# First-unit order of loads, TensorE, ScalarE and VectorE rewritten, with products of zeros ahead of the first scores

## The reference

```python
scores = scale * np.matmul(q, k.transpose(0, 1, 3, 2))          # batch 2, heads 8, seq 576, head_dim 64
mask_plain = (rel >= 0) & (rel < window)                        # window 32, heads 0..3
mask_dil = (rel >= 0) & (rel < window * dilation) & (rel % dilation == 0)
scores = scores - np.max(scores, axis=-1, keepdims=True)        # masked scores are -1e9
attn = np.exp(scores); attn = attn / (np.sum(attn, axis=-1, keepdims=True) + 1e-09)
x = np.matmul(attn, v)                                          # then as 1152 tokens x 512
for e in range(4):                                              # d_ff 1024
    out += p[:, e:e + 1] * (np.maximum(x @ w1[e], 0.0) @ w2[e])
h = out @ w_in                                                  # d_ff 2048
g = (a0 + a1*h + a2*h**2 + a3*h**3) / (1 + |b0||h| + |b1|h**2 + 1e-6)
return g @ w_out
```

## Time and profile before

| | us |
|---|---|
| median of 3 runs | 648.47 (646.71 to 650.09) |
| the profiled execution | 646.93 |
| its span, first to last instruction | 645.1 |
| PE busy | 633.8 |
| DVE / ACT / POOL busy | 387.2 / 319.1 / 268.9 |

### The profile page before, as it was taken

How to read it: one execution, slowest core, us unless ns; L and a number is a source line. 1 busy time by engine, 2 the same in 40 slices (tenths; PEclk the granted TensorE clock), 3 DMA queues, 4 the chain that set the end, 5 groups by cost and what they waited for, 6 DMA issues and landing times.

```text
span 645.1 us, 10644 instructions
## 1 busy us (share of the span) xinstructions
PE 633.8 (98%) x4004; PEld 563.4 (87%) x4004; DVE 387.2 (60%) x755; ACT 319.1 (49%) x742; POOL 268.9 (42%) x283
## 2 busy tenths in 40 slices
PE   6999999999999999999999999999999999999998
PEld 5788888988898889888898989889989998899996
DVE  4435352865665456234446325438988888889896
ACT  4874553333421343221443212336887777877774
POOL 4675112028860686300785100335722576732221
PEclk9999999999999999999999999999999999999999
DMA  9834220002130022100132100111530000001011
GB/s 305 260 92 131 62 73 1 2 33 67 66 98 2 34 99 98 34 2 1 42 109 80 33 1 1 59 41 49 162 149 1 1 0 2 2 0 50 2 49 50
DMA packets 20532, 37.68 MB, mean 58 GB/s; under 512 B 3392, under 2 KB 4032, under 8 KB 20480
## 3 DMA queue, kind: packets, MB, share of 16 engines
q1 hardware_dynamic: 20480, 36.99, 17.6%
HBM read 34.62 MB, written 2.36 MB: 57 GB/s over the span
## 4 chain that ended last, share of the span: by engine, by line
PE 94%; DMA 2%; ACT 1%; DVE 1%; issue 0%; SPq 0%; DVEq 0%; ACTq 0%
PE banks L739 46%; PE banks L655 24%; PE banks L713 20%; PE banks L627 2%; DMA scratch<-in_qk_dil 1%; PE banks L596 1%; PE banks L606 1%; DMA scratch<-in_qk_plain 1%; PE banks L775 1%; DVE h_lo L1262 0%; DVE acc L1168 0%; DVE acc L1163 0%; PE banks L615 0%; ACT scratch L856 0%; ACT w_hi L909 0%
## 5 line engine op out<-in xcount | busy, mean ns | idle before, releaser
L739 PE MATMUL banks<-w_hi,h_hi 128*128 128x512 f32 x432 | 171.6, 397 | 0.1
L739 PE MATMUL banks<-w_lo,h_hi 128*128 128x512 f32 x432 | 170.6, 395 | 0.0
L739 PE MATMUL banks<-w_hi,h_lo 128*128 128x512 f32 x429 | 169.9, 396 | 0.0
L1481 POOL TENSOR_TENSOR w_lo<-raw,w_hi 128x512 fp32r<-128x512 f32 x32 | 41.4, 1317 | 157.3 <-ACT w_hi L909 157.3
L655 PE MATMUL banks<-x_hi,w_hi 128*128 128x384 f32 (+1 forms) x320 | 104.9, 328 | 0.0
L655 PE MATMUL banks<-x_lo,w_hi 128*128 128x384 f32 (+1 forms) x320 | 102.5, 320 | 0.0
L655 PE MATMUL banks<-x_hi,w_lo 128*128 128x384 f32 (+1 forms) x320 | 102.3, 320 | 0.0
L1255 DVE TENSOR_TENSOR stage<-banks,stage 128x320 f32<-128x320 f32 (+1 forms) x120 | 54.1, 455 | 77.9 <-PE banks L713 75.0
L739 PEld LDWEIGHTS banks<-w_hi,h_lo 128*128 128x128 f32 x429 | 80.5, 188 | 19.3
L739 PEld LDWEIGHTS banks<-w_hi,h_hi 128*128 128x128 f32 x432 | 81.2, 188 | 14.6 <-issue 0.4
L739 PEld LDWEIGHTS banks<-w_lo,h_hi 128*128 128x128 f32 x432 | 81.2, 188 | 14.5
(11 more groups left out here) (116 smaller groups left out, 1240.4 us busy)
## 6 DMA issues: line engine op xcount, KB each, us to landing
raw<-in_weights SPq DMA_DIRECT2D x24, 512.0 KB, 3.6
raw<-in_weights SPq DMA_DIRECT2D x32, 256.0 KB, 2.7
raw_last<-in_weights SPq DMA_DIRECT2D x16, 256.0 KB, 5.5
scratch<-in_v SPq DMA_DIRECT2D x16, 192.0 KB, 4.0
scratch<-in_qk_dil SPq DMA_DIRECT2D x8, 320.0 KB, 5.2
out_t<-acc SPq DMA_DIRECT2D x9, 256.0 KB, 2.1
scratch<-in_qk_plain SPq DMA_DIRECT2D x8, 272.0 KB, 4.6
scratch<-in_qk_rest SPq DMA_DIRECT2D x2, 256.0 KB, 2.8
```

Source lines behind the costliest of these rows:

```text
L739: last = nc.tensor.matmul(sum_bank(k, t), h[:, cols], w[:, f, :], start=f == 0 and i == 0, stop=f == FC - 1 and i == 2)
L1481: last = nc.gpsimd.tensor_tensor(w1_lo[:, 2 * p + c].rearrange("p a b -> p (a b)"), raw1[:, c], w1_hi[:, 2 * p + c].rearrange("p a b -> p ...
```

## The change

All of it lies ahead of the steady loop, in the first unit.

- Loads: all query/key loads of blocks 0 to 3 come first, then all their value loads; the loads of blocks 4 to 7 are put among the eight weight loads. So `load_v(4)`, which waits for `values(0)`, stands ahead of `load_raw(4)`, and `load_v(5)` ahead of `load_raw(6)`. The three small loads (`prob`, `a_sb`, `b_sb`) come behind `load_v(7)`.
- PE: `fill` now multiplies a tile of zeros, which DVE sets in its first instruction, so it doesn't need the identity. Ten such products stand ahead of `scores(0)`, 28 more in five places (`FILLERS`); before there were 12 in three places. `turn(0)` comes ahead of `scores(4)`, and `values(3)` ahead of the whole `inner_product(0, 0)`. Chunks 1 and 3 are cut in two halves around a turn, not 3 to 1.
- DVE: block 0 is masked and reduced in two halves (`first_block`), so that ACT's exponentials of the first half can begin after the first. `mask(2)` comes ahead of `invert(0)`, and `mask(3)` ahead of `invert(1)`. DVE makes the high part of four inner weight chunks, no longer two.
- ACT: `exponentials(3)` comes ahead of `take_turned(1)`; `exponentials(4)` is no longer split around `attention_hi(2)` but stands behind `attention_hi(3)`; no `high_w1` ahead of `high(0, 0)`.

```diff
-FILLERS_FIRST = 4
-FILLERS = (3, 0, 5, 0)
+FILLERS = (10, 4, 12, 6, 3, 3)
...
-            def fill(w, n):
-
-                if w >= 2:
-                    pe.wait_ge(xa_lo, w - 1 if w < PAIRS else w)
+            def fill(bank, n):
+
                 for _ in range(n):
-                    nc.tensor.matmul(value_bank(w)[:, 0:P], ident[:, :], ident[:, :], start=True, stop=True)
+                    nc.tensor.matmul(bank[:, 0:P], zeros, zeros, start=True, stop=True)
...
+            pe.wait_ge(zeros_set, 1)
+            fill(turned_bank(0), FILLERS[0])
             scores(0)
...
-            def exponentials(w, part=None):
-                act.wait_ge(maxed, w + 1)
-                rows, part = soft_of(w), part or range(columns(w))
-                for n in part:
+            def exponentials(w):
+                if w == 0:
+                    act.wait_ge(first_maxed, 1)
+                else:
+                    act.wait_ge(maxed, w + 1)
+                rows = soft_of(w)
+                for n in range(columns(w)):
+                    if w == 0 and n == stacks(0):
+                        act.wait_ge(maxed, 1)
...
             def high_w1(c):
 
                 act.wait_ge(raw_in[c], 16)
+                act.wait_ge(w1_hi_done, 4)
...
+            def first_block():
+
+                dve.wait_ge(scored, 1)
+                dve.wait_ge(masks_made, 1)
+                m, n = start_mask.rearrange("p s c -> p (s c)"), stacks(0)
+                for half, done in ((0, first_maxed), (1, maxed)):
+                    part = slice(half * n, half * n + n)
+                    nc.vector.scalar_tensor_tensor(out=soft_of(0)[:, part, :].rearrange("p s c -> p (s c)"),
+                                                   in0=score_banks(0)[:, half, :], scalar=-SCALE, in1=m,
+                                                   op0=ALU.mult, op1=ALU.subtract)\
+                        .then_inc(first_masked if half == 0 else masked, 1)
...
+                    nc.vector.tensor_reduce(neg_max[:, 0, part], soft_of(0)[:, part, :], axis=AX.X, op=ALU.min)\
+                        .then_inc(done, 1)
...
+            nc.vector.memset(zeros, 0.0).then_inc(zeros_set, 1)
...
-            mask(0)
-            maximum(0)
+            first_block()
             mask(1)
             maximum(1)
+            mask(2)
             dve.wait_ge(small_set, 1)
             invert(0)
-            mask(2)
             maximum(2)
+            mask(3)
             invert(1)
-            mask(3)
             maximum(3)
```

More of the change, by code:

```diff
@@ L286, in build @@
         rest_mask = carve(TK)
+        zeros = carve(P)
         soft = carve(SOFT * 4 * TK).rearrange("p (s n c) -> p s n c", s=SOFT, c=TK)
@@ L313, in build @@
         prob_step = sem("prob_step")
+        zeros_set = sem("zeros_set")
         scored = sem("scored")
+        first_masked = sem("first_masked")
+        first_maxed = sem("first_maxed")
         masked = sem("masked")
@@ L528, in _ @@
                 load_qk(w)
-                if w:
-                    load_v(w - 1)
-            load_v(PAIRS - 1)
+            for w in range(PAIRS):
+                load_v(w)
+            load_raw(0)
             load_qk(PAIRS)
-            for c in range(FC):
-                load_raw(c)
-                if c == 2:
-                    load_qk(PAIRS + 1)
+            load_raw(1)
+            load_raw(2)
+            load_qk(PAIRS + 1)
+            load_raw(3)
+            load_v(PAIRS)
+            load_raw(4)
+            load_raw(5)
+            load_qk(PAIRS + 2)
+            load_v(PAIRS + 1)
+            load_raw(6)
+            load_raw(7)
+            load_qk(PAIRS + 3)
+            load_v(PAIRS + 2)
+            load_v(PAIRS + 3)
             sp.dma_start(prob[:, :, 0:MOE], probs).then_inc(prob_in, 16)
@@ L539, in _ @@
             sp.dma_start(b_sb[:, :], b.partition_broadcast(P)).then_inc(ab_in, 16)
-            for w in range(PAIRS, 2 * PAIRS):
-                if w >= PAIRS + 2:
-                    load_qk(w)
-                load_v(w)
             for w in range(2 * PAIRS, 3 * PAIRS):
@@ L777, in turn_x2 @@
                 last.then_inc(x2_turned, 1)
+            pe.wait_ge(zeros_set, 1)
+            fill(turned_bank(0), FILLERS[0])
             scores(0)
             scores(1)
-            pe.wait_ge(ident_made, 1)
-            fill(0, FILLERS_FIRST)
+            fill(turned_bank(0), FILLERS[1])
             scores(2)
             scores(3)
+            fill(turned_bank(0), FILLERS[2])
+            pe.wait_ge(ident_made, 1)
+            turn(0)
+            fill(turned_bank(1), FILLERS[3])
+            turn(1)
+            fill(value_bank(0), FILLERS[4])
+            values(0)
+            turn(2)
             scores(4)
-            turn(0)
-            turn(1)
-            fill(0, FILLERS[0])
-            values(0)
+            fill(value_bank(1), FILLERS[5])
             values(1)
-            turn(2)
-            fill(2, FILLERS[2])
+            turn(3)
             values(2)
-            turn(3)
-            inner_product(0, 0, range(DC - 1))
             values(3)
-            inner_product(0, 1, range(DC - 1))
-            inner_product(0, 0, range(DC - 1, DC))
+            inner_product(0, 0)
             scores(5)
+            inner_product(0, 1, range(0, 2))
             turn(4)
-            inner_product(0, 1, range(DC - 1, DC))
+            inner_product(0, 1, range(2, DC))
             values(4)
@@ L858, in exponentials @@
                                                 accum_out=row_sum[:, w % SOFT, n, 0:1])
-                if part[-1] == columns(w) - 1:
-                    last.then_inc(exped, 1)
+                last.then_inc(exped, 1)
             def take_turned(w):
```

35 lines of the change are left out of this document (18 added, 17 removed).

## The result

| | before | after |
|---|---|---|
| median of 5 runs | 649.41 us | 645.39 us |
| lowest to highest | 646.71 to 650.60 | 645.09 to 645.68 |
| profiled execution, its span | 646.93, 645.1 | 645.16, 643.4 |

The ratio is 0.9943, with a 95% interval of 0.9918 to 0.9967: 0.6% less, about as much as can be told from no change. The forecast was 646.4, in a range of 644.0 to 649.0. The two profiled executions differ by 1.77 us, the two medians by 4.0 us. Most of what follows is about what stands between these two numbers. The median of before is also 0.9 us higher than the 648.47 that the prediction started from; it had seen three of these five runs.

The account below looks back on a forecast made before the run. PE bounds the kernel, with time to win only in its first 31 us or so. 645.1 - 2.1 = 643.0 us of span, plus 1.83 gives 644.8 profiled; set against the median, 646.4 us, range 644.0 to 649.0.

Parts of the forecast that it names:

- walk: Following the written order engine by engine through the first unit: 1.9 us sooner at chunk 2, 2.2 at `values(5)`, 2.1 taken.
- What bounds it: PE, busy 633.8 of 645.1 us; time won up to about 31 us is kept if the other queues follow.
- The clock and the zeros: Ten zero products ahead of `scores(0)` raise PE's clock at 6.3 us, not 16.6, but delay `scores(0)` by 1.6 us.
- The rival in which zeros don't raise the clock: At the head, zero products leave PE's clock low and `turn(0)` comes at 15.9: slower, 651.2 us; chance 0.1.
- Halves: DVE's first block in halves: exponentials of block 0 gain 0.4 us, while block 1 waits 0.3 us longer.
- The weak place: Fillers hold `turn(0)` back 1.0 us, and `invert(1)` stands behind `mask(3)` with DVE idle; `values(0)` gains only 0.35 us.
- Loads at nothing: The moved loads of the first units are covered where wanted, by about 3 us, so they cost nothing.
- Without that cover 1.7 of the 2.1 us would go: If block 6's keys and values came as late as before, 1.7 of the 2.1 us gain would be lost.
- more than that: Rival at the head: earlier clock rise and sooner loads of blocks 2 and 3 give 2.8 us, 645.7 us; chance 0.17.
- The row with 0.1 us: DVE's fourth weight cast beside `normalise(4)`, ahead of `turn(4)`, costs 0.1 us; an exclusive port lock would cost 0.3.
- `low_w2` and POOL: `low_w2(0, 0)` on POOL ends at 30.35, just hidden behind scores 7 at 30.5; up to 0.5 us if ACT is late.
- From the profiled execution to the median: Profiled execution, forecast at 644.8 us, stands 1.54 below the median of 648.47, so the median forecast is 646.4 us.

Follow-up runs that it names:

- before + zeros: Kernel before with ten products of zeros put ahead of `scores(0)`, order and loads as before: 649.88 us, ratio 1.0024 against the kernel before.
- after without zeros: Kernel after without its ten leading products of zeros, the other 28 kept: 645.87 us, ratio 0.9962 against the kernel before.
- the old loads: Kernel after with the kernel before's order of loads, engines' orders as changed: 646.81 us, ratio 0.9976 against the kernel before.
- both, fewer still: Kernel after with `invert(1)` ahead of `mask(3)` and `FILLERS` (7, 3, 6, 4, 3, 3) for (10, 4, 12, 6, 3, 3): 643.16 us, ratio 0.9920 against before.
- before with the new loads: Kernel before with the kernel after's order of loads and nothing else: 647.40 us, ratio 0.9980 against the kernel before.
- before again: Kernel before, unchanged, run and profiled a second time: 648.12 us, ratio 0.9999 against the kernel before.

## Why the prediction was right or wrong, point by point

| mark | walk | before | after |
|---|---|---|---|
| scores 0 start | 5.4 | 3.83 | 5.17 |
| `turn(0)` | 11.45 | 12.25 | 11.08 |
| `turn(1)` | 13.9 | | 13.58 |
| `values(0)` | 15.05 | 15.40 | 14.83 |
| `values(1)` | 17.3 | | 17.37 |
| chunk 0 | 19.95 | | 20.15 |
| `turn(4)` | 23.2 | | 23.52 |
| chunk 2 | 25.6 | 27.37 | 25.95 |
| `values(5)` | 29.35 | 31.27 | 29.52 |

The columns before and after are of the first profiled executions. In the second one of the kernel after the clock rose at 6.7, and chunk 2 is at 26.75 and `values(5)` at 30.32.

- **What bounds it.** Right: what was won at 31 us, 1.75, was kept to the end: 1.7 us of span.
- **The clock and the zeros.** Right. The rise was at 4.6 in one execution and at 6.7 in the other, forecast at 6.3; `turn(0)` was at 11.08 and 11.88, forecast at 11.45, held by fillers each time. 2.1 us of rise moved it by 0.8, 0.38 for each us, where the prediction had 0.47. The rival in which zeros don't raise the clock is out. The rise stood 3.6 us into PE's run in one and 5.7 in the other, where the prediction took 5.2 from one trace.
- **Halves.** Exponentials 0 started at 6.58, before at 5.99: 0.6 us later, with scores 0 that start 1.3 us later. So halves and clock gave back 0.7 us, and the runs part the two. From the start of scores 0 to the start of exponentials 0 it took 2.16 us whole at the lower clock (before), 1.81 whole at the upper (before + zeros: 4.95 to 6.76), 1.75 in halves at the lower (after without zeros: 4.00 to 5.75) and 1.41 in halves at the upper (after). The halves are worth 0.4 us, as forecast, and the clock 0.35.
- **The walk.** 2.1 us was taken, 1.75 came at the second mark and 1.42 at the first. The term that was too small is PE's own work behind `values(0)`. From 14.83 to 18.56 it is unbroken, 3.7 us, where the walk gave 3.25 (15.05 to 18.3): 0.45 us that no engine's readiness explains. The walk took these stretches as if only the chain of softmax bound them; in the new order PE, with its fillers, does. By the second execution of the kernel after the gain is 0.6 and 0.95 us, since its clock rose later: the forecast's 2.1 is above both.
- **The weak place.** Right, and larger than written: DVE idle for 2.36 us, `invert(1)` behind it, worth 0.7 us by experiment; the fillers worth 1.1, where the walk had them hold `turn(0)` by 1.0. The two add.
- **Loads at nothing.** Right for the new order: PE waits for no load behind the first scores, and block 6's keys landed at 22.7, wanted at 25.46. "Without that cover 1.7 of the 2.1 us would go" was near in size, with 1.0 to 1.4 us by the medians. In the place it was half right: the wait that the old loads bring is that for the keys of block 3, and block 6's keys, landed at 26.7, are hidden behind it. The keys of blocks 2 and 3, sooner by what no longer stands ahead of them, were named in the rival of "more than that" and given no term in the sum.
- **Casts.** The row with 0.1 us was not the nearest case. One cast of the kernel after took 1.05 us, from 14.96, where others took 0.40 to 0.55. A low part of 1.27 us had begun on POOL at 14.46, and the normalisation that began at 15.69, while the cast still ran, took 1.01. In the variant "both, fewer still" a cast that began at 12.19, 0.07 us behind a normalisation, took 1.03, and the normalisation its usual 0.82. Each time the instruction that had begun first kept its time and the other grew. That agrees with the Trainium skill's rule of the shared port pair ("SBUF — State Buffer", section "SBUF: two separate sides"), by which the one that starts first gets the pair and the other blocks; whether this cast is of the kinds that the page names for it, no run shows. The fourth cast agrees in the order but not in the size: begun first, it took 0.40, and the normalisation beside it 0.92, 0.1 us more and not the whole 0.24 that the cast still had to run. The long cast is hidden here, as `attention_lo(0)` waited for ACT until 16.24; the 0.1 us is not, as `turn(4)` waits 0.28 us for that normalisation.
- **`low_w2` and POOL.** Right: the first outer product starts at 30.63, without a wait, 1.74 us sooner.
- **From the profiled execution to the median.** This is the step that failed. "That one is 1.54 below the median" was carried over as if it were noise that the change leaves alone. For the most part it was the clock: the 17 runs of before at full clock have a median of 646.88 and none above 648.92, and those at 0.996 or less one of 649.28. So of the three runs that the prediction had (646.71, 648.47, 650.09) the last very likely had falls; their clocks are not on record. The kernel after has none. Its profiled executions stand 0.23 below and 0.18 above the medians of their runs. With 0.23 for 1.54 the same sum would have given 645.0. The clue stood in the prediction, "the 3.4 us spread of the three runs", under the rival, and was not asked for its cause.
- **What was luck.** The number came within 1.0 us because two errors partly cancel: the walk promised 0.36 us too much (644.8 for the profiled execution, which took 645.16), and the way to the median put 1.31 too much on top (1.54 for 0.23). The range held the result, 645.39, mainly by the 1.6 us that were put into it as "luck in the runs", which was the steadier clock. "Faster by over 0.5%" had 0.2, and against the median of five runs, 649.41, it came to 0.57%.

## What to carry to other kernels

When a kernel's runs spread over more than the profiled execution explains, the spread is a term of the sum: look at the mean granted clock of every run to three places, and at PE's waits that come shortly ahead of dense work. An execution that is quicker at its head can end later, if it only comes sooner to a late load and waits there. A change that removes such waits can win twice, once their length and once the clock behind them. And fillers belong where PE would wait anyway: placed ahead of the step that the others wait for, or ahead of data that have landed, each costs 0.12 us an instruction at the full clock, and here a lead of zeros was worth nothing where later waits let the clock fall or where the work raised it soon enough itself.

## What the runs showed of the hardware

- Products of zeros raise TensorE's clock. With ten of them from 1.05 on, in seven profiled executions, it rose at about 4.2 to 7.2 us (4.2 in before + zeros, 4.6 and 6.7 in the two of the kernel after, 7.2 with the old loads). Without them it rose at 8.5 and 8.9 in two variants of the kernel after, at 8.5 in before with the new loads, and at 13.5 and 16.6 in the kernel before.
- The clock fell again four times in these traces, for 3.4 us each time, at 27.2 (before again), 11.0 and 28.1 (before + zeros) and 11.9 (before, new loads). Ahead of the falls PE had waited 1.54 and 0.70 us, 0.77 and 1.60, 1.80 and 1.17, and once 3.25. It did not fall behind a wait of 0.95 us in both, fewer still.
- A cast of 128 x 512 on DVE took 0.40 us to 1.05, the long ones beside an instruction of POOL that had begun before them.
- The same small load, `a_sb`, held SP for 8.82, 9.67 and 8.56 us with the old order of loads and for 2.83 and 2.89 with the new one. Why was not tried.
